# A mixture-of-experts layer: the narrow experts' second layer with split operands, activations stationary

## The reference

```
attention: 8 heads of 64, hash-bucket mask; x = its output, 768 x 512
expert_idx = argmax(x @ w_gate, axis=1)               # 8 experts, capacity 192 tokens each
h = maximum(einsum('ecd,edf->ecf', disp, w1), 0)      # 512 -> 1024
y = einsum('ecf,efd->ecd', h, w2)                     # 1024 -> 512
out[i] = gate_w[i] * y[expert_idx[i], pos[i]]
mish: h = out @ w_in (512 -> 2048); g = h * tanh(softplus(h)); g @ w_out (2048 -> 512)
```

## Time and profile before

| | us |
|---|---|
| Median of 3 runs (lowest, highest) | 402.27 (401.7, 402.83) |
| Profiled execution, span | 399.9 |
| PE busy in it | 392.4 |
| DVE, ACT, POOL busy | 242.7, 198.6, 90.5 |
| Granted TensorE clock | 1.000 |

### The profile page before, as it was taken

The page is one execution under the profiler, slowest core; times in us unless marked ns, Lnnn a source line. Parts: engine busy times, 40 slices in busy tenths (PEclk is TensorE's granted clock), DMA queues, the critical chain, the costliest instruction groups (busy, mean ns, idle before and its releaser), DMA issues.

```text
span 399.9 us, 7249 instructions
## 1 busy us (share of the span) xinstructions
PE 392.4 (98%) x2666; PEld 365.3 (91%) x2668; DVE 242.7 (61%) x407; ACT 198.6 (50%) x392; POOL 90.5 (23%) x96
## 2 busy tenths in 40 slices
PE   8999999999999999999999999999999999999995
PEld 3689999999999799999999999999889998899984
DVE  5888988988988612211110111049999998877761
ACT  6969779769888312110110110146676756544531
POOL 1942322320600150772464300000000000000015
PEclk9999999999999999999999999999999999999999
DMA  7675934964400348999999999600000000000004
GB/s 286 236 183 144 229 78 137 286 145 123 167 2 2 107 162 322 415 348 339 330 376 366 391 343 369 232 2 1 2 0 2 1 0 2 0 2 0 0 5 157
DMA packets 15803, 62.89 MB, mean 157 GB/s; under 512 B 2960, under 2 KB 3856, under 8 KB 11552
## 3 DMA queue, kind: packets, MB, share of 16 engines
q1 hardware_dynamic: 14272, 58.61, 43.6%
q0 software_dynamic: 992, 3.19, 2.1%
q10 hardware_dynamic: 512, 0.73, 0.6%
HBM read 49.89 MB, written 3.19 MB: 133 GB/s over the span
## 4 chain that ended last, share of the span: by engine, by line
PE 92%; DVE 2%; DMA 2%; SPq 1%; ACT 1%; issue 0%; POOLq 0%; POOL 0%; DVEq 0%
PE ps L880 17%; PE ps L905 16%; PE ps L802 15%; PE ps L820 14%; PE ps L697 8%; PE ps L725 7%; PE ps L606 7%; PE ps L680 3%; DMA raw<-in_kt 2%; PE ps L563 2%; PE ps L779 1%; PE ps L856 1%; DVE ptl L1277 1%; PE ps L567 1%; PE ps L738 1%
## 5 line engine op out<-in xcount | busy, mean ns | idle before, releaser
L802 PE MATMUL ps<-xs,ring 128*128 x512 | 60.0, 277 | 0.3
L802 PEld LDWEIGHTS ps<-xs,ring 128*128 128x128 f32 x512 | 58.7, 192 | 1.1 <-issue 1.1
L820 PE MATMUL ps<-hs,ring 128*128 128x128 f32 (+1 forms) x512 | 59.2, 276 | 0.0
L820 PEld LDWEIGHTS ps<-hs,ring 128*128 128x128 f32 x512 | 58.5, 192 | 0.0
L1030 ACT ACTIVATE pth<-ps 128x384 fp32r<-128x384 f32 x96 | 41.9, 490 | 20.1 <-PE ps L725 19.4
L1277 DVE TENSOR_TENSOR ptl<-ps,pth 128x384 fp32r<-128x384 f32 x96 | 48.9, 551 | 4.2 <-ACT pth L1030 3.3
L1220 DVE TENSOR_REDUCE nmax<-ps 128x1 f32<-128x768 f32 x48 | 45.6, 954 | 4.8 <-PE ps L606 2.7
L606 PE MATMUL ps<-ops 128*128 128x384 f32 x192 | 44.1, 351 | 0.2 <-ACT ops L954 0.2
L987 ACT ACTIVATE prob<-ps,nmax 128x768 f32<-128x768 f32 x48 | 43.5, 906 | 0.1
L880 PE MATMUL ps<-yh,wih 128*128 128x384 f32 x128 | 43.0, 336 | 0.0
L880 PE MATMUL ps<-yh,winlo 128*128 128x384 f32 x128 | 42.8, 335 | 0.0
(11 more groups left out here) (169 smaller groups left out, 683.4 us busy)
## 6 DMA issues: line engine op xcount, KB each, us to landing
ring<-in_w SPq DMA_DIRECT2D x32, 1024.0 KB, 7.8
winraw<-in_w_in SPq DMA_DIRECT2D x8, 512.0 KB
woutraw<-in_w_out SPq DMA_DIRECT2D x8, 512.0 KB
ops<-kh SPq DMA_DIRECT2D x12, 192.0 KB, 6.9
ops<-qh SPq DMA_DIRECT2D x6, 384.0 KB, 9.2
xg<-rows SPq DMA_DIRECT2D x1, 1539.0 KB, 6.4
raw<-in_vt SPq DMA_DIRECT2D x4, 384.0 KB, 4.9
raw<-in_qt SPq DMA_DIRECT2D x3, 384.0 KB, 6.2
```

The source lines that it names most:

```text
L802: last = mm(ps[:, fc // 2, (fc % 2) * WIDE:(fc % 2) * WIDE + W], wa[:, 2 * fc // KF, kd, P * (fc % (KF // 2)):P * (fc % (KF // 2)) + P], x ...
L820: last = mm(ps[:, 4 + half * KD // 2 + k, 0:W], wb[:, half, fc, P * k:P * k + P], hs[:, fc, 0:W], start=(fc == 0), stop=(fc == KF - 1))
```

## The change

In narrow experts the second layer changes sides. ACT writes the ReLU of two chunks to `hsh` (float32r) and then copies two chunks of w2 to `w2hi`; DVE writes the remainders `hsl` and `w2lo`. PE takes `hsh` and `hsl` as stationary operands and lets 512 columns of `w2hi` and `w2lo` move past, in one bank (YB): 8 x 3 float32r matmuls. The result stands with tokens on the partitions; ACT copies it to `ysb`, PE turns it with four transposes (`turn_rows`, bank YT) and ACT and DVE write `yh` and `yl` in one piece each. The turn of expert e is placed behind the first two chunks of expert e+1 where that is narrow, ahead of its first layer where it is wider, and ahead of the mish layers for the last. A wider expert keeps its float32 matmuls, in another order (output block outermost) and into banks 6 and 7; it waits for both halves of w2, and it raises the new count `w2l` by 4 at its end. An expert behind a wider one turns an old `ysb`, of which nothing is kept.

w2 is cut in DRAM by hidden chunk (two halves of four chunks) instead of by output column. SP loads a half of w2 when its split is done (`w2l`), between the halves of w1. `w2hi` and `w2lo` lie where the second half of the mish weights was loaded; that half (pieces 4 to 7, 4 MB) is now issued after the last expert, with a semaphore per piece, and GpSimd, ACT and DVE wait for the piece that they split. SP's loop is unrolled. In `up(0)` the terms with `yl` come last.

```diff
-        wb = ring[1][:, :].rearrange("p (h c n) -> p h c n", h=2, n=DM // 2)
+        wb = ring[1][:, :].rearrange("p (h c n) -> p h c n", h=2, n=DM)
...
+        top[0] = late + (KFF // 2) * KD * P * 4
+        w2hi = place("w2hi", [P, KF, DM], F32R)
+        top[0] = late + KFF * KD * P * 4 + (KFF // 2) * DM * 4
+        w2lo = place("w2lo", [P, KF, DM], F32R)
+        assert top[0] <= late + 2 * KFF * DM * 4
+        top[0] = d_base
+        hsh = place("hsh", [P, KF, NARROW], F32R)
+        hsl = place("hsl", [P, KF, NARROW], F32R)
+        ysb = place("ysb", [P, DM], F32)
...
+        YB, YT, SLOW = 4, 5, 6
+        EARLY = KFF // 2
+        XT_BANKS = (SLOW, SLOW + 1, 0, 1, 2, 3)
...
+                late_piece = str(piece) if 2 * piece >= EARLY else ""
+                sp.dma_start(winraw[:, at, :, :], w_in[:, at, :, :]).then_inc(s["wi" + late_piece], 16)
+                sp.dma_start(woutraw[:, at, :], w_out[:, at, :]).then_inc(s["wo" + late_piece], 16)
...
-            with sp.Fori(0, E - 1) as i:
+            for i in range(E - 1):
                 for half in range(2):
                     hold(sp, s["passed_sp"], s["Hw"], 4 * i + 2 * half + 2)
                     first_weights(i + 1, half)
-                hold(sp, s["passed_sp"], s["Yc"], i + 1)
-                second_weights(i + 1, 0)
-                hold(sp, s["passed_sp"], s["Yw"], i + 1)
-                second_weights(i + 1, 1)
-                hold(sp, s["passed_sp"], s["xt"], 6)
-                hold(sp, s["passed_sp"], s["wi"], 16 * i + 16)
-                hold(sp, s["passed_sp"], s["wo"], 16 * i + 16)
-                mish_weights(i + 1)
+                    hold(sp, s["passed_sp"], s["w2l"], 4 * i + 2 * half + 2)
+                    second_weights(i + 1, half)
+                if 2 * i + 4 <= EARLY:
+                    hold(sp, s["passed_sp"], s["xt"], 6)
+                    hold(sp, s["passed_sp"], s["wi"], 16 * i + 16)
+                    hold(sp, s["passed_sp"], s["wo"], 16 * i + 16)
+                    mish_weights(i + 1)
+            hold(sp, s["passed_sp"], s["Yw"], E)
+            for piece in range(EARLY // 2, KFF // 2):
+                mish_weights(piece)
...
+                def rows_in():
+
+                    pe.wait_ge(s["back"], 16)
+                    for b in XT_BANKS:
+                        for i in range(4):
+                            kd, t = xt_block(b, i)
+                            last = mm(ps[:, b, P * i:P * i + P], xg[:, t, P * kd:P * kd + P], c32("ident"),
+                                      is_transpose=True, start=True, stop=True)
+                        last.then_inc(s["xt"], 1)
...
+                def turn_rows(count):
+
+                    pe.wait_ge(s["ye"], count)
+                    for kd in range(KD):
+                        last = mm(ps[:, YT, P * kd:P * kd + P], ysb[:, P * kd:P * kd + P], c32("ident"),
+                                  is_transpose=True, start=True, stop=True)
+                    last.then_inc(s["Ty"], 1)
...
+                def narrow():
+
+                    first_layer(NARROW, range(2))
+                    with pe.If(e > 0):
+                        turn_rows(e + 1)
+                    first_layer(NARROW, range(2, KF))
+                    pe.wait_ge(s["ya"], 2 * e + 2)
+                    pe.wait_ge(s["yd"], 2 * e + 2)
+                    for fc in range(KF):
+                        if fc % 2 == 0:
+                            pe.wait_ge(s["Hd"], 2 + 4 * e + fc // 2 + 1)
+                            pe.wait_ge(s["w2l"], 4 * e + fc // 2 + 1)
+                        if fc == KF // 2:
+                            next_bounds()
+                        for n, (x, w) in enumerate(((hsh, w2hi), (hsh, w2lo), (hsl, w2hi))):
+                            last = mm(ps[:, YB, :], x[:, fc, :], w[:, fc, :], start=(fc == 0 and n == 0),
+                                      stop=(fc == KF - 1 and n == 2))
+                    last.then_inc(s["Yw"], 1)
+                    with pe.If(e < 1):
+                        rows_in()
+                    pe.nop()
...
+                def wider(W):
+
+                    first_layer(W, range(KF))
+                    pe.wait_ge(s["ya"], 2 * e + 2)
+                    pe.wait_ge(s["yd"], 2 * e + 2)
...
+                    for k in range(KD):
+                        if k == KD // 2:
+                            next_bounds()
...
+                    pe.wait_ge(s["Yw"], e + 1)
+                    pe.sem_inc(s["w2l"], 4)
...
+                    with pe.Else():
+                        turn_rows(e + 1)
...
-            pe.wait_ge(s["ya"], 2 * E + 1)
-            pe.wait_ge(s["yd"], 2 * E + 1)
+
+            turn_rows(E + 1)
+            pe.wait_ge(s["ya"], 2 * E + 2)
...
-                    terms = terms[:3 * KD // 2] + sorted(terms[3 * KD // 2:], key=lambda x: x[2] is yl)
+                    terms = sorted(terms, key=lambda x: x[2] is yl)
                 for c in range(2):
                     for n, (kd, w, y) in enumerate(terms):
-                        if f == 0 and c == 0 and n == 3 * KD // 2:
-                            pe.wait_ge(s["ya"], 2 * E + 2)
-                        if f == 0 and c == 0 and n == 3 * KD - KD // 2:
+                        if f == 0 and c == 0 and n == 2 * KD:
...
+                def narrow():
+
+                    for b in range(4):
+                        act.wait_ge(s["Hw"], 4 * e + b + 1)
+                        av(hsh[:, 2 * b:2 * b + 2, :],
+                           ps[:, b, 0:2 * WIDE].rearrange("p (a c) -> p a c", a=2)[:, :, 0:NARROW],
+                           ACT.Relu).then_inc(s["Ha"], 1)
+                        if b % 2 == 0:
+                            act.wait_ge(s[f"wb{b // 2}"], 16 * (e + 1))
+                        av(w2hi[:, 2 * b:2 * b + 2, :], wb[:, b // 2, 2 * (b % 2):2 * (b % 2) + 2, :],
+                           ACT.Copy).then_inc(s["w2h"], 1)
+                    act.wait_ge(s["Yw"], e + 1)
+                    av(ysb[:, :], ps[:, YB, :], ACT.Copy).then_inc(s["ye"], 1)
+                    with act.If(e < 1):
+                        rows_in()
+                    act.wait_ge(s["Ty"], e + 1)
+                    av(yh[:, :, bass.ds(st, NARROW)], ps[:, YT, :].rearrange("p (k c) -> p k c", k=KD),
+                       ACT.Copy).then_inc(s["ya"], 2)
+
+                def wider(W):
+
+                    act.sem_inc(s["w2h"], 4)
                     for b in (0, 2):
                         act.wait_ge(s["Hw"], 4 * e + b + 1)
                         av(hs[:, 2 * b:2 * b + 2, 0:W],
                            ps[:, b, 0:2 * WIDE].rearrange("p (a c) -> p a c", a=2)[:, :, 0:W],
-                           ACT.Relu).then_inc(s["Ha"], 1)
+                           ACT.Relu).then_inc(s["Ha"], 2)
+                    act.sem_inc(s["ye"], 1)
...
+                wait_mish(act, "wi", f)
...
+                def narrow():
+
+                    for b in range(4):
+                        dve.wait_ge(s["Ha"], 2 + 4 * e + b + 1)
+                        V.scalar_tensor_tensor(hsl[:, 2 * b:2 * b + 2, :],
+                                               ps[:, b, 0:2 * WIDE].rearrange("p (a c) -> p a c", a=2)[:, :, 0:NARROW],
+                                               0.0, hsh[:, 2 * b:2 * b + 2, :], ALU.max,
+                                               ALU.subtract).then_inc(s["Hd"], 1)
+                        dve.wait_ge(s["w2h"], 4 * e + b + 1)
+                        V.tensor_tensor(w2lo[:, 2 * b:2 * b + 2, :], wb[:, b // 2, 2 * (b % 2):2 * (b % 2) + 2, :],
+                                        w2hi[:, 2 * b:2 * b + 2, :], ALU.subtract).then_inc(s["w2l"], 1)
+                    with dve.If(e < 1):
+                        rows_in()
+                    dve.wait_ge(s["ya"], 2 * e + 4)
+                    V.tensor_tensor(yl[:, :, bass.ds(st, NARROW)], ps[:, YT, :].rearrange("p (k c) -> p k c", k=KD),
+                                    yh[:, :, bass.ds(st, NARROW)], ALU.subtract).then_inc(s["yd"], 2)
...
-              "w2": w2.reshape(E, F // P, P, 2, DM // 2).transpose(0, 3, 2, 1, 4),
+              "w2": w2.reshape(E, 2, F // P // 2, P, DM).transpose(0, 1, 3, 2, 4),
```

More of the change, by code:

```diff
@@ L134, in attention_moe_mish @@
         bounds = place("bounds", [P, E + 1, 2], I32)
-        mark = place("mark", [P, 4], F32)
+        mark = place("mark", [P, 5], F32)
         toki = place("toki", [P, NT], U32)
@@ L310, in attention_moe_mish, with wait_mish, xt_block @@
         SHORT = WIDE // NT
+        YB, YT, SLOW = 4, 5, 6
+        EARLY = KFF // 2
+        XT_BANKS = (SLOW, SLOW + 1, 0, 1, 2, 3)
+        def wait_mish(e, name, f):
+            piece = f // 2
+            if f < EARLY:
+                e.wait_ge(s[name], 16 * (piece + 1))
+            else:
+                e.wait_ge(s[f"{name}{piece}"], 16)
+        def xt_block(b, i):
+            return (2 * (b - SLOW) + i // 2, 4 + i % 2) if b >= SLOW else (b, i)
         def by_slot(first_kd, end_kd, many):
```

(30 more changed lines are left out.)

102 lines of the change are left out of this document (44 added, 58 removed).

## The result

| | before | after |
|---|---|---|
| Median (lowest, highest), us | 402.1 (401.7, 402.8) | 415.4 (414.3, 416.7) |
| Ratio, 95% interval | | 1.033 (1.031 to 1.035) |
| Span of the profiled execution, us | 399.9 | 412.2 |

A forecast was written before the change was run, and what follows sets the result against it. PE, busy in 98% of the span, was taken as the bound. Terms -11.55 + 3.7 + 1.65 + 1.1 + 2.15 + 0.4 + 5.7 = +3.15 gave span 403.05; with 2.37 for the median, 405.4 us, range 401.0 to 410.0.

The forecast's parts named there:

- experts 4 to 7 at -4.8: Last four narrow experts: shorter second layer (-1.65 us each) and added turn (+0.46 each), forecast -4.8 us in all.
- the wider expert at +1.6: Expert 2: PE waits 1.1 us for the copy before the turn, plus 0.46 for the turn, forecast +1.6 us.
- w1 half 1 of expert 1 landing at 165.7: Expert 1: this load queues behind w2 half 0 and lands at 165.7; PE wants it at 165.3, so +0.4 us.
- The end: Before the first mish matmul: PE waits for two copies (1.1 and 1.05 us) and turns (0.46), forecast +2.6 us.
- D: Narrow second layers: matmul steps wait for DVE (1.65 against 1.37 us per step), 407 us; chance 16% shared with B.
- A: Expert 3, faster: w1 half 1 lands within 5.6 us of issue, stall under 2.3; 400.0 with none; chance 22%.
- B: Narrow experts: weights pace them too, 1 us for each of experts 4 to 7, 409.4 us; chance 16% shared with D.
- expert 1 at -0.8: Expert 1: -1.65 us for the shorter second layer, +0.46 for the turn, +0.4 for waiting on w1 half 1.
- Expert 0 gains nothing: Expert 0: ACT's late first ReLU delays the four remainder steps, cancelling the second layer's gain, +1.65 us against the list.
- the late half of the mish weights is not waited for: Mish layers: the 4 MB issued after the last expert arrive in some 14 us, up(8) 54 us on; no stall.
- rival C: Start of mish layers: GpSimd's splits of f = 8 and 9 and DVE delay each other, 3 us, 408.4; chance 12%.
- the stall of 5.4 us in expert 3: Expert 3: w1 half 1, issued only after the wider expert, lands at E + 9.8; PE stalls 5.4 us (3.0 to 8.2).

## Why the prediction was wrong

**What held.** 24 matmuls in 5.50 us (5.49); the turn at 0.46 (0.44, behind a wait 0.66); ACT's and DVE's 128x1024 operations at 1.07 and 1.22 (means of 1055 and 1268 ns); experts 4 to 7 at -4.8 (-4.9); the wider expert at +1.6 (+1.4); w1 half 1 of expert 1 landing at 165.7 (165.0 with the code moved, though by other terms: issued at 151.06, it took 13.94 us). The end came out at 2.1 for 2.6: its waits for copies are 0.7 and 0.8 us instead of 1.1 and 1.05, because ACT's 0.38 us were counted from PE's last issue, whereas PE's list runs to the end of that matmul (issued at 157.64 in expert 0, ended at 158.03, ACT at 158.07). Of the rivals, D fell. A fell on its landing (6.86 us where it needed under 5.6); its other sign, a stall under 2.3 us, did appear (1.5), but only because PE had already stood 1.75 us in its wait for itself. B fell for the changed kernel (experts 4 to 7 run at 13.07 each); with the code moved 0.9 us was lost there, 0.6 of it in one wait for a load.

**The step that failed first: expert 1 at -0.8.** It came out at +5.6. The sum priced what PE executes and what it waits for, and took the code as always there, a term put at nothing without a reason, though the rewritten bodies are those that PE branches between. A gap of 4.27 us, the 1.6 us that the lower clock costs in the 16 records behind it, and an `hsl` that came 0.9 late make 6.8, in place of the 0.4 us for w1 half 1. Moved by 200 slots the same instructions give +0.2. With the gap in expert 0 the code's place accounts for 7.5 us of the 13.3, and no rival had it. That the place does it is shown by the two runs with another offset; that the engine waits for a fetch of code is the likely reason, not shown.

**"Expert 0 gains nothing" was right by accident.** It was argued from ACT's first ReLU at 148.07, 5.0 us behind PE's start. With the code moved that ReLU starts at 145.46, 2.1 us behind PE's start, ACT and DVE keep pace, and expert 0 gains 1.5 us. The late row was taken for a property of the work, and was one of that one program; what made ACT late in it wasn't looked into. In the changed kernel PE's own gap of 1.78 us took the gain.

**The second: GpSimd and DVE.** The step that the late half of the mish weights is not waited for is literally true; no trace shows PE waiting for them. What it moved along was GpSimd's work. This was rival C, priced at 3 us and given 12%; it is 5.1 here, 5.8 alone and 4.9 when taken away. That "nothing says that they collide" was a poor reason to leave out a term: the rows of before only failed to show it, because they had no such overlap. The Trainium skill's rule that the prediction cited ("SBUF — State Buffer", section "SBUF: two separate sides") is borne out in direction: the operations of both engines lengthen (DVE's 0.56 to 1.63, GpSimd's cast 0.61 to 0.94). The estimate fell short since it looked at `down(0)` alone, with its margin of 3.6 us. `gl` of f = 0 starts 17.2 us behind the first mish matmul, before 12.0, so DVE is 5.1 late, and `down(0)` stands for 0.9 and 1.0 us; but `up(4)` and `up(5)`, for which the prediction counted no margin, then stand another 0.4 and 1.5 us for `hc`.

**The third, with the other sign: the stall of 5.4 us in expert 3.** It measured 1.5, plus 1.75 marked issue where I had put 0.3 for PE's wait for itself, a term that no row of before gives, so 3.3 for 5.7. (The row moved by 2.0 only, since the records behind each of the two waits take some 0.27 us longer: 16 in 2.05 for 1.78, 32 in 3.84 for 3.57.) The load was issued 0.6 us behind the wider expert's end, not 1.1, and landed 6.9 us after its issue, not 8.7. It was the second of a pair as in the earlier trace rows, but I had misread that pair as uncongested: two loads of 192 KB had been issued 1.1 us ahead of it, and here nothing was. The spare transpose showed the 1.75 to be the price of the wait.

Without the code's place and the collision, the kernel is at 403.3 by experiment; the forecast of 405.4, corrected for expert 3 (-2.0), is 403.4. So close an agreement is luck: in that run's trace experts 0 and 1 together are 1.4 us above the forecast and the end 0.5 below, and the runs lie 1.8 us above the span where 2.37 was taken. The range was wrong because it took in sizes of known steps only.

Left open: the rule by which a code place brings a gap, why the gaps differ between 1.8 and 7.7 us, and how much of expert 1's late `hsl` comes from GpSimd's splits beside DVE there (`w2lo` took up to 1.98 us, GpSimd's casts up to 1.62 and its subtractions up to 2.06) and how much from the gap; no run took those splits alone away.

## What to carry to other kernels

When an edit rewrites a body that an engine branches to, run it at two or three code offsets before you judge it: here the place alone was worth 7.5 us in one kernel and about 8 in the other, more than any other loss of this edit. When work is moved in time, list which engine's other work it will now stand beside, and price DVE beside GpSimd as if one waited for the other. And don't let an engine wait for its own last instruction to raise a count; let an instruction raise it.

## What the runs showed of the hardware

- A gap of PE can cost twice: 4.27 us of standstill, then 16 records in 3.38 us for 1.79, at a granted clock of 0.58. Gaps of about 2 us left 0.56 in one kernel (1.99 us, row transposes moved) and 1.00 in two others (1.75 and 2.04 us).
- The same instructions took 415.4 or 407.9 us by their place, and 427.9 with two bodies swapped.
- GpSimd beside DVE lengthened DVE's TENSOR_SCALAR with one source of 128x384 from 0.36 to 1.45 us, not only operations with two SBUF sources (0.56 to 1.63).
- A float32r matmul of 128x512 steps at 0.229 us also with weights and activations swapped (24 in 5.49).
- PE waiting for its own count stood still 1.74 to 2.04 us in eight kernels; a spare transpose in its place left no gap.
